# The first channel product of batches 1 to 3 by Strassen's method, in an attention and mixer kernel

## What is computed

```python
# q, k, v: (4, 8, 576, 64); w_tok1 (576, 256); w_tok2 (256, 576); w_ch1 (512, 1536); w_ch2 (1536, 512); all fp32
q_rot, k_rot = rotate(q), rotate(k)
scores = 1 / sqrt(64) * matmul(q_rot, k_rot.transpose(0, 1, 3, 2))
attn = exp(scores - max(scores)); attn = attn / (sum(attn) + 1e-09)
x = matmul(attn, v).transpose(0, 2, 1, 3).reshape(4, 576, 512)
h = maximum(x.transpose(0, 2, 1) @ w_tok1, 0) @ w_tok2
u = x + h.transpose(0, 2, 1)
out = u + maximum(u @ w_ch1, 0) @ w_ch2
```

## Time and profile before

| | before |
|---|---|
| median of 3 runs (lowest to highest) | 657.23 us (657.11 to 657.34) |
| the profiled execution's own time | 656.14 us |
| its span, first to last instruction | 654.3 us |
| mean granted TensorE clock | 0.998 |
| PE, DVE, ACT, POOL busy | 97%, 71%, 63%, 39% |
| one batch on PE (u units of batch 1 to those of batch 2; 2 to 3) | 89.1 us; 88.6 us |

### The profile page before, as it was taken

How to read it: one execution, slowest core, us unless ns; L and a number is a source line. 1 busy time by engine, 2 the same in 40 slices (tenths; PEclk the granted TensorE clock), 3 DMA queues, 4 the chain that set the end, 5 groups by cost and what they waited for, 6 DMA issues and landing times.

```text
span 654.3 us, 13564 instructions
## 1 busy us (share of the span) xinstructions
PE 635.7 (97%) x4832; PEld 618.9 (95%) x4832; DVE 461.6 (71%) x825; ACT 413.7 (63%) x923; POOL 254.6 (39%) x253
## 2 busy tenths in 40 slices
PE   3899999999999999999999999999999999999997
PEld 2799999999999999999999999999999999999997
DVE  7899999999999999877476852238820387413485
ACT  4888999988888899875555542336532255423353
POOL 3998999988888885554600000000000000000000
PEclk9999999999999999999999999999999999999999
DMA  4576767666678764316000310000310002100002
GB/s 134 123 176 182 206 157 177 174 177 179 170 183 216 198 177 118 90 29 201 2 1 2 82 52 21 1 1 2 99 55 0 0 0 80 72 1 2 1 2 72
DMA packets 60408, 59.16 MB, mean 90 GB/s; under 512 B 18752, under 2 KB 46016, under 8 KB 60352
## 3 DMA queue, kind: packets, MB, share of 16 engines
q1 hardware_dynamic: 59904, 58.32, 33.0%
q10 hardware_dynamic: 448, 0.10, 0.1%
HBM read 28.31 MB, written 9.44 MB: 58 GB/s over the span
## 4 chain that ended last, share of the span: by engine, by line
PE 93%; DVE 2%; ACT 1%; DMA 1%; issue 1%; SPq 1%; ACTq 0%; DVEq 0%
PE slot L596 12%; PE rest L629 12%; PE rest L606 9%; PE slot L1245 8%; PE slot L1243 8%; PE slot L1244 8%; PE rest L1245 6%; PE rest L1243 6%; PE rest L1244 6%; PE rest L361 3%; PE rest L558 3%; PE rest L616 2%; PE slot L1275 2%; PE rest L1275 2%; PE rest L218 1%; PE rest L215 1%
## 5 line engine op out<-in xcount | busy, mean ns | idle before, releaser
L1517 DVE TENSOR_TENSOR pieces<-h,pieces 128x288 fp32r<-128x288 f32 x168 | 75.0, 453 | 88.6 <-ACT pieces L1431 88.3
L963 DVE TENSOR_REDUCE neg_max<-slot 128x1 f32<-128x576 f32 x142 | 106.5, 751 | 6.7 <-PE slot L596 2.0
L1431 ACT ACTIVATE pieces<-h 128x288 fp32r<-128x288 f32 x168 | 74.5, 444 | 46.4 <-PE slot L1245 28.3
L971 DVE TENSOR_TENSOR pt_lo<-rest,pt_hi 128x512 fp32r<-128x512 f32 x144 | 95.8, 676 | 1.9 <-ACT pt_hi L827 1.4
L629 PE MATMUL rest<-pt_hi,v 128*128 128x256 f32 (+1 forms) x320 | 89.3, 303 | 0.0
L827 ACT ACTIVATE pt_hi<-rest 128x512 fp32r<-128x512 f32 x144 | 84.0, 595 | 4.7 <-PE rest L606 4.1
L629 PE MATMUL rest<-pt_lo,v 128*128 128x256 f32 (+1 forms) x256 | 69.7, 295 | 0.0
L596 PE MATMUL slot<-key,q_hi 128*128 128x288 f32 x252 | 63.3, 332 | 3.0 <-ACT q_hi L866 1.5
L820 ACT ACTIVATE prob_a<-slot,neg_max 128x576 f32<-128x576 f32 x78 | 58.0, 743 | 10.4 <-DVE neg_max L963 10.1
L629 PEld LDWEIGHTS rest<-pt_hi,v 128*128 128x128 f32 x320 | 60.3, 188 | 0.2
L1530 DVE TENSOR_TENSOR h<-h 128x288 f32<-128x288 f32 x96 | 41.5, 451 | 24.8 <-ACT h L1413 24.4
(11 more groups left out here) (198 smaller groups left out, 1912.5 us busy)
## 6 DMA issues: line engine op xcount, KB each, us to landing
key<-t_hi_k SPq DMA_DIRECT2D x30, 144.0 KB, 2.3
key<-t_lo_k SPq DMA_DIRECT2D x30, 144.0 KB, 2.4
raw_qk<-in_q_dram SPq DMA_DIRECT2D x16, 256.0 KB, 2.9
raw_v<-in_v_dram SPq DMA_DIRECT2D x16, 256.0 KB, 3.2
x_scratch<-x_pair SPq DMA_DIRECT2D x16, 256.0 KB, 2.3
stage_or_x<-x_scratch SPq DMA_DIRECT2D x16, 256.0 KB, 3.7
raw_qk<-in_k_dram SPq DMA_DIRECT2D x15, 256.0 KB, 2.8
q_hi<-t_hi_q SPq DMA_DIRECT2D x30, 128.0 KB, 2.4
```

The costliest lines, as they stand in the source:

```text
L963: dve.tensor_reduce(neg_max[p % 2][:, i:i + 1], slot[g if 2 <= g < 4 else g % 2][:, :, 0:HALF], AX.XY, ALU.max, negate=True).then_inc(maxe ...
L971: dve.tensor_tensor(pt_lo[:, :, cols], rest[:, bank, :].rearrange("p (j n) -> p j n", j=G), f32(pt_hi[:, 0:G, cols]), ALU.subtract).then_i ...
L1431: act.activation(pieces[:, ring(m), 0, :], source[WEIGHTS[n]][:, ft, :], ACT.Copy).then_inc(piece_hi, 1)
L1517: dve.tensor_tensor(pieces[:, ring(m), 1, :], source[WEIGHTS[n]][:, ft, :], f32(pieces[:, ring(m), 0, :]), ALU.subtract).then_inc(piece_lo, 1)
```

## The change

Batches 1 to 3 make the hidden stage from 7 products of half the contraction, each of 3 units of 12 matmuls (21 units, `shared`), in the order A11, S2, S3, A22, A12, S1, S4 of the weight's shares. Batch 0 keeps its 12 units. What comes with it:

- w_ch1 is loaded a second time, in fp32, over `wc1`, once batch 0 has its last unit of h: four DMAs of 768 KB. POOL makes the sums S1 to S4 from it, four operations of 128x1536, during batch 0's channel stage.
- The parts of the weights aren't kept: for each of the 21 units of a batch ACT makes hi (`ring_part`, 128x512) and POOL makes lo (`ring_rest`, 128x512) in a ring of three, three units ahead.
- u is kept in fp32 (`u_whole`, ACT); DVE makes four sums of its quarters (`share_sum`, 128x576), and for each product ACT and DVE make the parts of the right operand (`share_part`, `share_rest`, 128x576) in two buffers. DVE's 8 operations of `u_lo` and two of `add_u` are gone in these batches.
- Running sums stay in the PSUM slots; C11 and C22 are kept by ACT and C12 by DVE (`keep`). A unit of C11, C22 and C12 is finished by DVE with two operations, an addition from PSUM and a maximum in place that waits for the addition (`c_out`); C21 by ACT. C12 is now the last quarter.
- In the attention phase `token.split_hi(act, 0, 0)` stands a few instructions earlier in ACT's queue.

```diff
@@ build
+            w1_sums = sb(placed, "w_ch1_sums", [P, 7, CT // 2, CH // 2])
+            w1_parts = [sb(placed, f"w_ch1_part_{n}", [P, CT // 2, 2 * P], F32R) for n in range(3)]
@@ attention, scalar
+            if p == N - 1:
+                act.wait_ge(products, 4 * N)
+                token.split_hi(act, 0, 0)
             exponent(p, 1)
...
-            if p == N - 1:
-                act.wait_ge(products, 4 * N)
-                token.split_hi(act, 0, 0)
@@ mixer
+    SHARES = ("A11", "S2", "S3", "A22", "A12", "S1", "S4")
+    PAIR = HF // 2
+    def ring_unit(k):
+        if k % 3 == 0:
+            return w1_parts[0], w1_parts[1]
+        if k % 3 == 1:
+            return w1_parts[2], free_piece
+        if k < LATER:
+            return h_early[:, 8:10, 0:2 * P], h_early[:, 10:12, 0:2 * P]
+        return t2_t3[:, 0], t2_t3[:, 1]
@@ sync
+            sp.wait_ge(done["C22"], PAIR)
+            for name, c, n in (("S3", u_low, half[1]), ("A22", u_high, half[1]), ("A11", u_low, half[0]), ("A12", u_high, half[0])):
+                sp.dma_start(share[name], w[:, c, n]).then_inc(w1_in, 16)
@@ gpsimd
+        pool.wait_ge(w1_in, 4 * 16)
+        share_sum("S1", "S3", "A22", ALU.add)
+        pool.wait_ge(w1_s_done, 1)
+        share_sum("S2", "S1", "A11", ALU.subtract)
+        share_sum("S3", "A11", "S3", ALU.subtract)
+        pool.wait_ge(w1_s_done, 3)
+        share_sum("S4", "A12", "S2", ALU.subtract)
+        def ring_rest(b, k):
+            n, i = divmod(k, PAIR)
+            pool.wait_ge(ring_hi, (b - 1) * HIDDEN + k + 1)
+            hi, lo = ring_unit(k)
+            pool.tensor_tensor(lo[:], share[SHARES[n]][:, :, 2 * i * P:2 * (i + 1) * P], f32(hi[:]), ALU.subtract).then_inc(ring_lo, 1)
+        with pool.Fori(1, B) as b:
+            for k in range(HIDDEN):
+                ring_rest(b, k)
@@ tensor
+        def shared(b, n, i):
...
+            elif name == "S3":
+                pe.wait_ge(kept["S2"], (b - 1) * PAIR + i + 1)
...
+            elif name == "S1":
+                if i == 0:
+                    pe.wait_ge(done["C21"], b * PAIR + PAIR)
+                else:
+                    pe.wait_ge(done["C11"], b * PAIR + (1 if i == 1 else 3))
+            else:
+                pe.wait_ge(done["C22"], b * PAIR + i + 1)
+            if i == 0:
+                pe.wait_ge(share_lo, (b - 1) * len(SHARES) + n + 1)
+            pe.wait_ge(ring_lo, (b - 1) * HIDDEN + k + 1)
+            unit, x = ring_unit(k), u_parts[n % 2]
+            for c in range(CT // 2):
+                for g in range(2):
+                    mm = products(s[:, g, 0:HALF], [w[:, c, g * P:(g + 1) * P] for w in unit],
+                                  [x[:, a, c, :] for a in range(2)], c == 0 and name in ("A11", "A12", "S1"), c == CT // 2 - 1)
@@ scalar
+            for n, name in enumerate(SHARES):
+                for i in range(PAIR):
+                    k = n * PAIR + i + 3
+                    if k < HIDDEN:
+                        ring_part(b, k)
+                    if i == 0 and n + 1 < len(SHARES):
+                        share_part(b, n + 1)
+                    if name in ("A11", "S3"):
+                        keep(b, name, i)
+                    elif name == "A22":
+                        c21_out(b, i)
...
             if not last:
+                ring_part(b + 1, 0, first_batch=begins)
@@ vector
+        def c_out(b, name, of, i):
...
+            dve.tensor_tensor(part, share_slot(of, i)[:, :, 0:HALF], part, ALU.add).then_inc(c_added, 1)
+            dve.wait_ge(c_added, (b - 1) * 3 * PAIR + order + 1)
+            dve.tensor_scalar(part, part, 0.0, None, ALU.max).then_inc(done[name], 1)
+        def shares(b):
+            share_sum(b, 0, u[:, u_low, right], u[:, u_low, left], 2)
+            share_rest(b, 0)
+            share_sum(b, 1, u[:, u_high, right], sums[0], CT)
+            share_sum(b, 2, u[:, u_high, right], u[:, u_low, right], CT)
+            share_rest(b, 1)
+            share_sum(b, 3, u[:, u_high, left], sums[1], CT)
+            share_rest(b, 2)
+            for i in range(PAIR):
+                keep(b, i)
+            share_rest(b, 3)
+            share_rest(b, 4)
+            share_rest(b, 5)
+            c_out(b, "C11", "A12", 0)
+            c_out(b, "C11", "A12", 1)
+            c_out(b, "C11", "A12", 2)
+            share_rest(b, 6)
+            for i in range(PAIR):
+                c_out(b, "C22", "S1", i)
+            c_out(b, "C12", "S4", 0)
+            los(b, 0, 2)
+            c_out(b, "C12", "S4", 1)
+            lo(b, 2)
+            c_out(b, "C12", "S4", 2)
...
-            los(b, 0, 3)
-            add_u(b, 0)
+                los(b, 0, 3)
+                add_u(b, 0)
+            else:
+                shares(b)
             lo(b, 3)
             t1(b, 0)
```

More of the change, by code:

```diff
@@ L107, in build @@
         with ExitStack() as ctx:
-            then = mixer(nc, ctx, sb, slot, ident, h, h1, pieces, token, wt2, wc1, w1, x_stored, first, w_ch2, out)
+            then = mixer(nc, ctx, sb, slot, ident, h, h1, pieces, token, wt2, wc1, w1, w1_sums, w1_parts, h_early, x_stored, first, w_ch1, w_ch2,
+                         out)
             with nc.Block() as block:
@@ L1107, in attention, with mixer @@
                  last_store=last_store, buffers_left=buffers_left, values_left=values_left, slot_left=slot_left)
-def mixer(nc, ctx, sb, slot, ident, h, h1, pieces, token, wt2, wc1, w1, x_stored, first, w_ch2, out):
+def mixer(nc, ctx, sb, slot, ident, h, h1, pieces, token, wt2, wc1, w1, w1_sums, w1_parts, h_early, x_stored, first, w_ch1, w_ch2,
+          out):
     def sem(name):
@@ L1169, in mixer @@
     O11, O12, O21, O22 = ((c, t) for c in (c_top, c_low) for t in (left, right))
-    w_in = sem("w_ch2_in")
+    share = {name: w1_sums[:, n] for n, name in enumerate(SHARES)}
+    u_low, u_high, sums = slice(0, CT // 2), slice(CT // 2, CT), [out_t[:, i, :].rearrange("p (c n) -> p c n", c=2) for i in range(4)]
+    right_of = {"A11": u[:, u_low, left], "S2": sums[1], "S3": sums[2], "A22": sums[3], "A12": u[:, u_high, left], "S1": sums[0],
+                "S4": u[:, u_high, right]}
+    u_parts = [pieces[:].rearrange("p r a n -> p (r a n)")[:, (1 + 2 * i) * 2 * HALF:(3 + 2 * i) * 2 * HALF]
+               .rearrange("p (a c n) -> p a c n", a=2, c=2) for i in range(2)]
+    free_piece = pieces[:, 0].rearrange("p a n -> p (a n)")[:, 0:4 * P].rearrange("p (c n) -> p c n", c=2)
+    t2_t3 = ut[1][:, 1:3, :].rearrange("p a n -> p (a n)")[:, 0:8 * P].rearrange("p (a c n) -> p a c n", a=2, c=2)
+    LATER = 11
+    quarter = {"C11": (top, left), "C12": (top, right), "C21": (low, left), "C22": (low, right)}
+    w_in = sem("w_ch2_in")
+    w1_in, w1_s_done, ring_hi, ring_lo = sem("w_ch1_in"), sem("w_ch1_sums_done"), sem("ring_hi"), sem("ring_lo")
+    share_t, share_hi, share_lo = sem("share_t"), sem("share_hi"), sem("share_lo")
+    kept = {name: sem(f"kept_{name}") for name in ("A11", "S2", "S3")}
+    c_added = sem("c_added")
+    done = {name: sem(f"{name}_done") for name in quarter}
     s_done, w2_hi_done, w2_lo_done = sem("w_ch2_sums_done"), sem("w_ch2_hi_done"), sem("w_ch2_lo_done")
@@ L1367, in body @@
                     first.last_o(pe)
-            for j in range(HIDDEN):
-                hidden(b, j, begins)
+            if begins:
+                for j in range(PLAIN):
+                    hidden(j)
+            else:
+                for n in range(len(SHARES)):
+                    for i in range(PAIR):
+                        shared(b, n, i)
             for n in range(len(WEIGHTS) - 1):
@@ new lines, in ring_part @@
+        def ring_part(b, k, first_batch=False):
+            n, i = divmod(k, PAIR)
+            if k == 0 and first_batch:
+                act.wait_ge(w1_in, 4 * 16)
+            elif k == 1:
+                ready(act, b, 1)
+            elif k == 2:
+                for r in range(3):
+                    act.wait_ge(stored[r], b * STORES[r])
+            elif k >= 3:
+                ready(act, b, CT + k - 2)
+            if k == LATER:
+                act.wait_ge(share_t, (b - 1) * 4 + 4)
+                act.wait_ge(share_lo, (b - 1) * len(SHARES) + 3)
+            if k == PAIR:
+                act.wait_ge(w1_s_done, 4)
+            act.activation(ring_unit(k)[0][:], share[SHARES[n]][:, :, 2 * i * P:2 * (i + 1) * P], ACT.Copy).then_inc(ring_hi, 1)
@@ L1427, in hi @@
             if n in (0, 2, 5):
-                act.wait_ge(h_done, b * HIDDEN + {0: 3, 2: 6, 5: 12}[n])
+                act.wait_ge(done[{0: "C11", 2: "C21", 5: "C22"}[n]], b * PAIR + PAIR)
             else:
```

175 lines of the change are left out of this document (132 added, 43 removed).

## The result

The changed kernel takes 678.48 us (median of 4 runs, 677.33 to 679.33) against 657.20 before: the ratio is 1.032, with a 95% interval of 1.0305 to 1.034. The forecast was 682 us, in a range of 663 to 691. The profiled execution has a span of 676.6 us against 654.3, 22.3 more, on 108 matmuls fewer.

A forecast was written before the change was run, and what follows sets the result against it. PE, busy for 97% of the span, was taken as the bound. Terms: -14.4 + 25.2 + 12.6 + 0.9 + 1.0 = +25.3 us on the median of 657.23, giving 682 us, range 663 to 691.

The forecast's parts named there:

- the likeliest case: Wherever POOL and DVE both work within SBUF: each waits for the other's whole operation, turn by turn; 682 us, chance 0.55.
- the signs named: Among them: PE idle for two stretches of 5 us and more; in batches 1 to 3 waits before pieces 3, 5, 6.
- Matmuls: Hidden stage, batches 1 to 3: 36 matmuls fewer per batch, 4.80 us each batch, -14.4 us in three.
- Batch 0: Batch 0's channel stage: DVE takes turns with POOL's sums, piece 19 comes late, +12.6 us; slower PE clock, +0.9.
- the lighter rival: DVE works in bursts, POOL gets the gaps; batch 0 loses 4.7 us, total +11.1, 668 us (663 to 674); chance 0.25.
- Hidden stage: Batches 1 to 3: PE waits 0.8, 1.55 and 2.5 us before units 6, 17 and 18, 4.85 us a batch.
- my two bounds: DVE's maximum in place on 576 elements: between 0.37 and 0.67 us, the middle, 0.52, taken.
- Channel stage: Batches 1 to 3: PE waits 0.8, 0.3, 2.15, 0.3 us for lo(3) to lo(6), 3.55 a batch; x parts 0.5 in two batches.
- the rival at 694: Waits of 2 us and more also slow PE's pace, 1.7 us in three batches, more in batch 0; 694 us, chance 0.03.
- Attention phase: Moving a split up in ACT's queue issues the same instruction and no DMA: 0 us, bounds -0.6 and +0.6.
- the faster one: No collision in short operations, maximum 0.37 us; only the channel stage's head waits, 2.8 us; -6.0, 651 us (650 to 656), chance 0.12.
- "no gain, no loss" rival: No collision, but the maximum takes 0.67 us: hidden 0.6, channel 4.15, together 4.75 of 4.80 us; 657 us, chance 0.05.

The follow-up runs named there:

- the run with zeros: Changed kernel with POOL's four sums of w_ch1 left out, POOL writing zeros over the same elements in two operations at the same point: 667.4 us.
- one difference behind each lo: Changed kernel with DVE's 24 differences reordered, in batches 1 to 3 one ahead of each lo from lo(6) on: 679.7 us, 1.036 times the kernel before.

## Why the prediction was right

**Direction and size** held, 678.5 against 682, and the mechanism of the likeliest case, one whole operation of each in turn, is what the runs show once POOL has come in. Of the signs named, two failed: PE was never idle for 5 us at a stretch (2.6 at most), and it waited before pieces 3, 4 and 5, but not before 6. Term by term:

- *Matmuls*, -14.4: the count fell by 108, from 4832 to 4724.
- *Batch 0*, 12.6 and 0.9: 12.5 by the start of batch 1, 12.0 by the run with zeros. The course was a mixture. DVE did run at full pace with POOL waiting, as the lighter rival had it, from 358.9 to 362.1; but at its first gap the turns began as the forecast had them. By then its differences were done, so that each turn gave PE a piece, and not every second one. The turns cost 9.5 us, less than the 12.6, and the clock 2.7, more than the 0.9: the two errors nearly cancel, which is luck.
- *Hidden stage*, 4.85 a batch: 3.0 measured (44.80 against 41.76). This was too much. I had 0.8, 1.55 and 2.5 us before units 6, 17 and 18. PE's recorded waits were 0.4, 0.9 and 0.4, and 0.25 more before unit 19. Most of the error is in the last term: `share_rest` 6 was to wait for POOL's unit 19, but came 0.06 us ahead of an operation of POOL, and C22's first maximum took 0.76 and not a whole turn. The maximum took 0.46 by itself, so 0.37 or so from start to start, the lower of my two bounds and not the middle; C11's three waited only 0.3 to 0.4 us each, for the tail of an operation of POOL.
- *Channel stage*, 3.55 and 0.5 for the x parts: 5.7 measured. This was too little. By the starts of matmuls pieces 3, 4 and 5 came 0.4, 0.2 and 2.05 us late in batch 2 (the wait for lo(5) is 1.89 on record, 2.15 by the working), together 2.6 and so under 3.55. The rows waited 1.0 (0.7 on average). What was missing is the clock: 1.5 us behind the wait for lo(5) in each of the three batches. I had it as part of the rival at 694, with a chance of 0.03. Waits, rows and clock make 5.1 of the 5.7; the rest is not told apart.
- *Attention phase*, 0: the u units of batch 0 start within 0.8 us of before in all kernels, early or late; no difference to be told.

The two errors in batches 1 to 3, 1.8 down and 1.6 up in batch 2, nearly cancel; the sum was right in part by that. Of the rivals, the run without the ring's lo parts tests the faster one in batches 1 to 3: it gains 0.15 us in batch 2 and not 2.0, so even without collisions there would have been next to no gain. For the "no gain, no loss" rival that is nearly its number, for another reason than the one given (the maximum at 0.67): the maximum took 0.46, and the clock behind lo(5) took the rest.

The rule of the Trainium skill on the exclusive lock, page "SBUF — State Buffer", section "SBUF: two separate sides", holds in what collides and for how long: two sources in SBUF collide, a source in PSUM doesn't, and by the run with zeros POOL does not hold DVE off when it only writes. The Trainium skill limits there the lock of a two-source operation to a GpSimd operation that reads SBUF, and the run with zeros agrees. That whichever starts first gets the port fits `share_rest` 6, but is not the whole of it: POOL's first sum had begun at 358.92, and eight of DVE's operations that began later went ahead of it, 24 with the one difference behind each lo. The rule of the Trainium skill, page "VectorE: DVE Perf Modes", section "The perf-mode tier table", that a one-source fp32 operation runs at twice the rate, holds too: 460 ns for 576 elements against 750 with two sources.

## What to carry to other kernels

Work moved to GpSimd is not free while VectorE has two-source operations within SBUF to do: count what stands behind each of them, and put long GpSimd operations where VectorE reads PSUM or rests, or cut them up. A reduction of matmuls is lost where the engine that feeds the next stage finishes later than before; here the product that ends the hidden stage decided which differences came last, and their order in one queue was worth 12 us. Where a queue alternates two kinds of work with another engine between them, keep the producer two or more steps ahead of its reader.

## What the runs showed of the hardware that I had not expected

- An unbroken run of VectorE operations keeps a waiting GpSimd operation out: 3.1 us for a sum of 3.5 us (record of 6.58), 2.9 us for a piece of 0.59 (record of 3.52), and 9.1 us for a sum where the run was longer (record of 12.64). It ended at a gap of 0.16 us, or at an operation of VectorE that reads PSUM. Once GpSimd is in, they take turns one by one. Why a long run is not broken into and a blocked one is stays open; no run here tells it.
- The granted clock fell to its lower level behind a single wait of 1.9 us, in 4 us with PE half busy (0.57 in the next stretch), in each of batches 1 to 3, at about 1.5 us each; through the four sums in batch 0 it stayed there (0.50). Four waits of 0.3 us in a row, in the run with one difference behind each lo from lo(6) on, left it at 1.00. So the long wait cost more than its length, and the short ones did not.
